# Attention and two token/channel mixers on one core: plain first pair in each chunk, attention's tail takes over splits

## The reference

```python
# attention, B=2, H=8, S=768, D=64, 16 clusters: q and k meet only where
# their nearest centroids agree
scores = np.where(mask, scale * (q @ k.T), -1e9)
x = softmax(scores) @ v                       # -> (B, S, 512)
# mixer 1: U (768,32), V (32,768), w_ch1 (512,2048), w_ch2 (2048,512)
u = x + (x.T @ U @ V).T
x = u + relu(u @ w_ch1) @ w_ch2
# mixer 2: w_tok1 (768,256), w_tok2 (256,768), w_ch1 (512,1536), w_ch2 (1536,512)
u = x + (relu(x.T @ w_tok1) @ w_tok2).T
out = u + relu(u @ w_ch1) @ w_ch2             # (2, 768, 512) float32
```

## Time and profile before

| | us |
|---|---|
| median of 3 runs | 819.98 (818.78 to 821.72) |
| the profiled execution | 820.13 |
| its span, first to last instruction | 818.2 |
| PE busy in the span | 767.1 (94%) |
| DVE, ACT, POOL busy | 579.1, 386.0, 234.2 |
| mean granted clock of TensorE | 0.97 |

### The profile page before, as it was taken

How to read it: one execution, slowest core, us unless ns; L and a number is a source line. 1 busy time by engine, 2 the same in 40 slices (tenths; PEclk the granted TensorE clock), 3 DMA queues, 4 the chain that set the end, 5 groups by cost and what they waited for, 6 DMA issues and landing times.

```text
span 818.2 us, 12517 instructions
## 1 busy us (share of the span) xinstructions
PE 767.1 (94%) x4165; PEld 684.9 (84%) x4165; DVE 579.1 (71%) x893; ACT 386.0 (47%) x698; POOL 234.2 (29%) x262
## 2 busy tenths in 40 slices
PE   7989999999999757999999799999979999979998
PEld 6878999999998546888888588888868898868987
DVE  5678999999998897556558656556694556585554
ACT  5568888888886532232236322232450242442320
POOL 1342233223348881221112511221051221103100
PEclk9999999999999967999999899999998999999999
DMA  8935444443530402212210112212110212033002
GB/s 252 203 107 141 98 120 110 106 119 98 127 89 1 155 26 78 78 52 67 88 52 1 52 52 78 78 52 68 35 52 28 76 52 78 26 131 100 27 26 77
DMA packets 64042, 66.64 MB, mean 81 GB/s; under 512 B 6400, under 2 KB 53824, under 8 KB 64000
## 3 DMA queue, kind: packets, MB, share of 16 engines
q1 hardware_dynamic: 64000, 66.09, 28.9%
HBM read 42.27 MB, written 4.72 MB: 57 GB/s over the span
## 4 chain that ended last, share of the span: by engine, by line
PE 56%; DVE 8%; issue 3%; POOL 0%; ACT 0%; ACTq 0%
PE bank L1101 28%; PE bank L1087 23%; PE bank L1053 3%; DVE bc_lo L1279 2%; DVE h L1299 1%; PE bank L1069 1%; DVE a_lo L1245 1%; DVE kT_hi L1303 1%; DVE x L1258 1%; DVE x L1253 1%; DVE moving_sum L1273 1%; PE bank L1038 0%; POOL kT_hi L979 0%; DVE w_lo L1284 0%; DVE kT_hi L1289 0%
## 5 line engine op out<-in xcount | busy, mean ns | idle before, releaser
L1182 ACT ACTIVATE qT_hi<-h 128x768 fp32r<-128x768 f32 x56 | 47.4, 846 | 303.8 <-DVE h L1299 245.1
L1087 PE MATMUL bank<-bc_hi,a_hi 128*128 128x384 f32 x392 | 136.1, 347 | 18.2 <-DVE bc_lo L1279 12.8
L1087 PE MATMUL bank<-bc_lo,a_hi 128*128 128x384 f32 x392 | 135.3, 345 | 0.0
L1087 PE MATMUL bank<-bc_hi,a_lo 128*128 128x384 f32 x392 | 134.4, 343 | 0.0
L1101 PE MATMUL bank<-w_hi,kT_hi 128*128 128x512 f32 x336 | 133.7, 398 | 0.0
L1101 PE MATMUL bank<-w_lo,qT_hi 128*128 128x512 f32 x336 | 133.0, 396 | 0.0
L1101 PE MATMUL bank<-w_hi,qT_hi 128*128 128x512 f32 x336 | 132.6, 395 | 0.0
L1299 DVE TENSOR_TENSOR h<-bank,h 128x384 f32<-128x384 f32 x140 | 75.0, 552 | 51.3 <-PE bank L1087 51.2
L969 POOL TENSOR_TENSOR a_raw<-a_raw 128x256 f32<-128x256 f32 x28 | 24.3, 868 | 285.1 <-DMA a_raw<-in_moe_w_ch_dram 285.1
L1289 DVE SCALAR_TENSOR_TENSOR kT_hi<-h,qT_hi 128x768 fp32r<-128x768 f32 x56 | 59.4, 1061 | 64.6 <-ACT qT_hi L1182 64.6
L595 DVE TENSOR_TENSOR pT_lo<-back,pT_hi 128x384 fp32r<-128x384 f32 x192 | 98.0, 551 | 6.7 <-ACT pT_hi L496 3.3
(11 more groups left out here) (144 smaller groups left out, 1380.1 us busy)
## 6 DMA issues: line engine op xcount, KB each, us to landing
a_raw<-in_moe_w_ch_dram SPq DMA_DIRECT2D x56, 256.0 KB, 3.2
w_raw<-in_moe_w_ch_dram SPq DMA_DIRECT2D x56, 256.0 KB, 2.7
Q<-qT_hi SPq DMA_DIRECT2D x64, 96.0 KB, 2.2
K<-kT_hi SPq DMA_DIRECT2D x64, 96.0 KB, 2.1
q_raw<-in_q_dram SPq DMA_DIRECT2D x8, 384.0 KB, 5.8
k_raw<-in_k_dram SPq DMA_DIRECT2D x8, 384.0 KB, 6.7
Q<-qT_lo SPq DMA_DIRECT2D x32, 96.0 KB, 2.1
K<-kT_lo SPq DMA_DIRECT2D x32, 96.0 KB, 2.1
```

Source lines behind the costliest of these rows:

```text
L1087: last = nc.tensor.matmul(up_bank(n, q), w[n % 2][:, A_SLOT[q], kt, :], y[:, q, kt, :], start=(kt == 0 and i == 0), stop=(kt == 1 and i == 2))
L1182: nc.scalar.activation(hs_hi[:, e, :], h[:, e, :], ACT.Relu).then_inc(hs_hi_made, 1)
```

## The change

The first pair of each chunk no longer uses the seven products. It is computed as four groups (i, k), one for each half of h. A group is 12 matmuls of 384 columns into one bank (`group`), over the plain blocks of the weights and of the tokens. ACT and DVE apply relu and split straight from that bank (`group_high`, `group_low`). The plain token blocks are split straight from the bank of the transposition (`block_high` on ACT, `block_low` on DVE), before `uT_copy` copies the tile to uT. The sums over uT and their splits (`t_block`, `t_high`, `t_low`) are needed only from pair 1 on. The first pairs need no `pair_sums`.

In attention, GpSimd splits three token tiles of sequence 0 in each of the pairs 5 and 6. In the last pair it splits U, V, and the columns of the first three head pairs of the six tiles of sequence 1. SP loads the weights of the pairs 0 and 1 once the last heads are in. PE ends attention with the 12 matmuls of the first token product of sequence 0. The mixers' block then only splits the last 128 columns of the six tiles of sequence 1. The loads and splits of wt1 and wt2 move from its start into the pairs 1 and 2 of chunk 0. In mixed chunks `token_second` moves behind product 1 of pair 1. The temporaries of the sums lie in h, and the raw token weights in uT.

```diff
@@ attention, SP: at the end
+            for j in range(2):
+                sp.wait_ge(head_in[j], NPAIR * HEAD_LOADS)
+            w3 = w_ch1.rearrange("(k p) f -> p k f", p=P)
+            for n in range(2):
+                for i in range(2):
+                    sp.dma_start(a_raw[n][:, 2 * i:2 * i + 2, :, :].rearrange("p s k c -> p (s k) c"),
+                                 w3[:, :, (2 * n + i) * P:(2 * n + i + 1) * P]).then_inc(w1_in[n], 16)
@@ attention, GpSimd
...
                     if last_pair:
                         if G == 0:
+                            for j in range(2):
+                                pool.wait_ge(head_in[j], NPAIR * HEAD_LOADS)
                             pool.wait_ge(uv_in, 5 * 16)
                             split_U()
-                        for i in range(2 * G, min(2 * G + 2, NT)):
-                            split_x(i)
+                        elif G == 1:
+                            split_V()
+                        else:
+                            if G == 2:
+                                pool.wait_ge(x_done, (NPAIR - 1) * GPP)
+                            for i in range(GT * (G - 2), GT * (G - 1)):
+                                split_x(1, i)
@@ attention, PE: at the end
+            U_st = q_lo[:, 0, :].rearrange("p (t c) -> p t c", t=NT)
+            pe.wait_ge(exp_done, NPAIR * TPP)
+            pe.wait_ge(U_split, 4)
+            pe.wait_ge(x0_split, 2 * NT)
+            for t in range(NT):
+                for n in range(2):
+                    last = nc.tensor.matmul(front[:, 0:DM], U_st[:, t, :], token_tiles(hi[n])[:, t, :],
+                                            start=(t == 0 and n == 0), stop=(t == NT - 1 and n == 1))
+            last.then_inc(tok_mm, 1)
@@ mixers, PE
+            def group(cc, g):
+
+                n, (i, k) = pbase[cc], GROUPS[g]
+                pe.wait_ge(b_made, cc * NT + NT // 2 * (k + 1))
+                if g == 0:
+                    pe.wait_ge(a_made, 2 * (n + 1))
+                if g < 2:
+                    pe.wait_ge(uT_made, cc * NT + (g + 1 if cc == 0 else NT - 1 + g))
+                else:
+                    pe.wait_ge(group_made, 4 * cc + g - 1)
+                for j in range(2):
+                    for kt in range(2):
+                        for c, (w, y) in enumerate(((a_hi, bc_hi), (a_hi, bc_lo), (a_lo, bc_hi))):
+                            last = nc.tensor.matmul(ring_bank(cc, g)[:, 0:GW], w[n % 2][:, 2 * i + j, kt, :],
+                                                    y[:, 5 * k + j, kt, :], start=(j == 0 and kt == 0 and c == 0),
+                                                    stop=(j == 1 and kt == 1 and c == 2))
+                last.then_inc(group_mm, 1)
...
             for cc in range(NCH):
-                for p in range(npair[cc]):
-                    for q in range(PRODS):
+                for g in range(len(GROUPS)):
+                    if cc == 0 and g < 2:
+                        for t in range(GT):
+                            transpose_u(0, GT * g + t)
+                    group(cc, g)
+                    if cc == 0 and g > 0:
+                        for t in range(2 * g - 2, 2 * g):
+                            token_second_low(1, t)
+                    if cc in MIXED:
+                        for t in ((), (0,), (1, 2), (3, 4, 5))[g]:
+                            token_first(cc, t)
+                for p in range(1, npair[cc]):
+                    for q in range(BLOCKS):
                         product(cc, p, q)
+                        if cc in MIXED and p == 1 and q == 1:
+                            for t in range(NT):
+                                token_second(cc, t)
@@ mixers, ACT
+            def block_high(cc, t):
+                act.wait_ge(u_tr, cc * NT + t + 1)
+                nc.scalar.activation(split_tile(bc_hi, t), turned(cc, t), ACT.Copy).then_inc(b_hi_made, 1)
+
             def uT_copy(cc, t):
-                act.wait_ge(u_tr, cc * NT + t + 1)
...
+                act.wait_ge(b_made, cc * NT + t + 1)
+                nc.scalar.activation(uT[:, :, t * P:(t + 1) * P], turned(cc, t), ACT.Copy).then_inc(uT_made, 1)
...
+                else:
+                    for t in range(NT):
+                        block_high(cc, t)
+                        if t > 0:
+                            uT_copy(cc, t - 1)
+                    uT_copy(cc, NT - 1)
...
+                    t_high(cc, 0)
+                    t_high(cc, 1)
+                    group_high(cc, 0)
+                    a_high(n + 1)
+                    t_high(cc, 2)
+                    group_high(cc, 1)
@@ mixers, DVE
+                dve.wait_ge(uT_made, NT * (cc + 1))
+                t_block(tmp2, block_of(0, 1), block_of(0, 0))
+                dve.wait_ge(t_sum, 4 * cc + 1)
+                t_block(tmp1, block_of(1, 1), tmp2)
+                t_block(block_of(0, 1), block_of(1, 1), block_of(0, 1))
...
+                    t_low(cc, 0)
+                    t_low(cc, 1)
+                    group_low(cc, 0)
+                    for part in range(2):
+                        a_low(n + 1, part)
+                    t_low(cc, 2)
+                    group_low(cc, 1)
+                    settle(cc, 0)
+                    settle(cc, 1)
+                    w2_low(n)
+                    group_low(cc, 2)
+                    settle(cc, 2)
+                    settle(cc, 3)
+                dve.wait_ge(t_made, 4 * cc + 1)
+                t_block(tmp1, block_of(1, 0), tmp1)
+                group_low(cc, 3)
+                if not mixed:
+                    settle(cc, 4)
+                    settle(cc, 5)
+                t_low(cc, 3)
```

More of the change, by code:

```diff
@@ new lines, in _ @@
+                for half in range(2):
+                    for t in range(GT * half, GT * half + GT):
+                        if cc == 0:
+                            add_mix(0, t)
+                    for t in range(GT * half, GT * half + GT):
+                        block_low(cc, t)
+                dve.wait_ge(uT_made, NT * (cc + 1))
+                t_block(tmp2, block_of(0, 1), block_of(0, 0))
+                dve.wait_ge(t_sum, 4 * cc + 1)
+                t_block(tmp1, block_of(1, 1), tmp2)
@@ new lines, in _ @@
+                dve.wait_ge(t_made, 4 * cc + 1)
[5 more added lines that the diff above has]
+                t_low(cc, 3)
+                if mixed:
+                    for r in range(NR):
+                        t2_low(cc, r)
+                for n in range(pbase[cc] + 1, pbase[cc + 1]):
+                    more = n + 1 < PAIRS_ALL
+                    combine(n, 1, c11, snap)
+                    if mixed and n == pbase[cc] + 1:
```

559 lines of the change are left out of this document (292 added, 267 removed).

## The result

| | before | after |
|---|---|---|
| median (lowest to highest, runs) | 820.63 us (818.78 to 821.72, 4) | 806.98 us (805.07 to 808.34, 4) |
| the profiled execution, its span | 820.13, 818.2 | 807.81, 806.0 |
| PE busy, mean granted clock | 767.1, 0.970 | 760.1, 0.989 |

The ratio is 0.9834, with a 95% interval of 0.9805 to 0.9864. The kernel is 13.7 us faster; the forecast was 806.0.

The account below looks back on a forecast made before the run. A steady-state pair was taken as bound by PE: its matmul columns, waits and clock. Terms of 11.7 (start and pair 1), 2.0, 2.0 and -1.6 summed to 14.1 off 820.13, giving 806.0 us, range 801 to 810.

Parts of the forecast that it names:

- Part 1: First pair of each chunk: four groups of 12 matmuls, 48 instead of 42, +1.04 us in each of four chunks.
- Part 2: Attention's last pair: GpSimd's added splits fit with 0.5 us slack, taken as 0; mixers start at 269.3 instead of 268.2.
- the list of signs: Trace marks for right or wrong; wrong included attention ending after 267 or chunk 0's first group later than 284.
- Part 3: Start of chunk 0: first down unit at 307.5 against 318.22, a gain of 10.7 us; 11.7 with pair 1.
- pair 1's loss at half clock: Chunk 0, pair 1: it had lost 2.1 us at half clock; 1.0 of that was kept as gain.
- the term that I priced 0: Chunk 0, pairs 1 and 2: wt1 and wt2 splits, 11 us on GpSimd beside VectorE work, cost nothing.
- Part 4: Transposition ring, chunks 1 to 3: 1.93 us a step, so downs end 4.0 us later at each of three boundaries.
- the rival: Clock falls in the transposition ring: 2.9 us lost at each of three boundaries, 814.7 us in all; chance 0.22.
- Part 5: After the ring: chunk 3 gains 2.4, chunks 1 and 2 6.0 each; less 4.0, a 1.6 loss and 2.0 gains.
- The sum: Whole kernel: 11.7 + 2.0 + 2.0 - 1.6 = 14.1 us faster, giving 806.0.

Follow-up runs that it names:

- changed again: The changed kernel itself, unedited, profiled a second time in another session; its span was 803.7 us, against 806.0 in the first profile.
- e2: Changed kernel with GpSimd splitting the second half of w_tok2 one pair later, in pair 3 of chunk 0; 804.69 us against 806.98.
- e9: Changed kernel with the edits of e1_ring and e2 together, without the other order of the blocks; 797.85 us against 806.98.
- e1_ring: Changed kernel with ScalarE copying each transposed tile right behind its high part, bank freed after VectorE's low part, chunks 1 to 3; 801.01 us against 806.98.
- e5: Changed kernel with VectorE doing additions and group low parts earlier in chunks 0 and 3, and sums pair 1 needs later; 809.13 us against 806.98.

## Why the prediction was right, point by point

**Part 1, the work of a group.** The 12 matmuls of group 0 in chunk 3 take 2.12 us in the chain, as two products do. Right.

**Part 2, attention's end.** Right, at a slack that was hardly larger than told (GpSimd's last finishes, with the idle time ahead):

```profile
265.02 0.82 POOL L410 TENSOR_TENSOR qT_hi<-x,zero 128x384 fp32r<-128x384 f32 x1
265.92 1.01 POOL L413 TENSOR_TENSOR kT_hi<-x,qT_hi 128x384 fp32r<-128x384 f32 x1
...
269.05 0.60 POOL L394 TENSOR_TENSOR avsum<-av 128x192 f32<-128x192 f32 x1 [0.92 <-ACT av L537]
```

A narrow tile takes 1.86, for which I had 1.9, and GpSimd idles 0.92 us before the last finish. Attention's own length is 202.82 against 202.86. That it ended 2.4 later in this execution came from the stretch ahead of it. By the list of signs this ("attention ending after 267", "a first group later than 284") would have stood for wrong: it was 268.5 and 284.3, for a reason that lies ahead of what was changed. A sign should be a distance between two marks, not a place in the span.

**Part 3, chunk 0.** The step that was mis-sized. From attention's last copy (266.08 before) I had the first group after 16.2 us and the first down unit after 41.4; three executions whose clock stayed up in the token product (changed again, e2, e9) have 14.2 and 37.5, the profiled one 15.8 and 39.4. The gain of this stretch was thus 12.7, and 14.6 in those three, where 10.7 was told. PE in the profiled execution:

```profile
284.32 0.44 PE L1157 MATMUL bank<-bc_hi,a_hi 128*128 128x384 f32 x1 [1.73 <-DVE bc_lo L1395]
...
289.36 0.41 PE L1157 MATMUL bank<-bc_hi,a_hi 128*128 128x384 f32 x1 [1.37 <-ACT uT L1259]
...
296.51 0.66 PE L1157 MATMUL bank<-bc_hi,a_hi 128*128 128x384 f32 x1 [3.91 <-DVE kT_hi L1411]
...
307.89 0.39 PE L1193 MATMUL bank<-w_hi,qT_hi 128*128 128x512 f32 x1
```

Two terms were too high in all four. The low part of the 768 late columns took 1.47 and not 1.9. And of the groups 2 and 3, group 2 alone ran at 1.2 GHz, behind the 3.91 us wait that I had foreseen, while group 3 was back at 2.4 GHz. The 12 matmuls of sequence 1's token product took the 4.1 told there, and 2.9 in "changed, again" (272.91 to 275.77). The stretches of sequence 1's token product, of group 2 and of what follows it:

```profile
273.90:281.10 7.20, 7.18 (x24) 5.70 (x25) 4.45 (x6) 0.60 (x1) 2.23 (x2) 0.76 0.20 69
...
296.50:301.00 4.50, 4.18 (x12) 3.68 (x12) 4.10 (x6) 2.79 (x6) 0.00 (x0) 0.50 0.00 0
301.00:305.00 4.00, 3.92 (x17) 3.62 (x18) 4.00 (x7) 0.22 (x1) 0.00 (x0) 0.80 0.38 128
```

The first of them is what separates the executions: in this one the clock fell to 1.2 GHz amid the token product (0.76 over the stretch). In "changed, again", at the same place, it didn't:

```profile
272.90:280.10 7.20, 7.05 (x36) 5.79 (x36) 5.25 (x7) 1.57 (x3) 2.22 (x2) 1.00 0.40 125
```

The wait ahead of it is the same 2.71 us in both. Which of the two a run gets isn't settled by anything I measured; it costs 1.6 us ahead of the first group here, and 2.9 in e1_ring (0.57 over its token product).

I had kept 1.0 of pair 1's loss at half clock. All of it went: 13.72 us from unit 0 to the next pair, where it was 15.6.

The error on the other side is the term that I priced 0: the wt2 splits beside VectorE's low parts. I had allowed for a doubling and found 0.4 us to spare. I had also put the splits of wt1 and wt2 at 11 us together; GpSimd was busy 6.2 us with the first and 9.4 with the second in the changed kernel. w2_low took 3.37 instead of 1.28 and a_low's first part 3.26 instead of 1.21, 2.6 and 2.7 times as much, and pair 2 took 17.23 us (321.61 to 338.84 in the chain) instead of the 15.6 that a pair takes. That is the +1.6 that e2 took away. The Trainium skill (SBUF — State Buffer, "Who interferes with whom") says that a VectorE instruction with two inputs in SBUF contends with a GpSimd instruction that reads SBUF, and that the one which comes second is blocked until the other is through. The trace agrees. a_low starts at 329.93 beside a GpSimd operation that ends at 332.11 (329.53 + 2.58); 332.11 plus its lone 1.21 is 333.3, and it ended at 333.19. w2_low is two instructions. The first meets the last 0.8 us of the 2.25 operation, the second, which the chain has at 327.89, the last 1.6 us of the CAST; 1.28 + 0.8 + 1.6 is 3.7, and it took 3.37. So what is added is the rest of the GpSimd operation that is met, and a doubling was the wrong picture of it.

**Part 4, the ring.** Right in mechanism and size. A step took 1.89 (1.93 told), T2 waited 1.74 (about 2 told), T0 to T5 took 9.15 instead of 5.23, +3.9 (4.0 told), all of it on the path (e1). The waits before T3 to T5 show as 0.58 and not 0.8 to 0.9, since the modelled end of a matmul lies past the start of the next work. The clock is the rival's point. The three rings of the changed kernel (boundaries 3, 2 and 1):

```profile
688.00:698.00 10.00, 6.53 (x40) 4.63 (x38) 4.37 (x7) 5.67 (x10) 0.27 (x1) 1.00 0.00 0
568.00:578.00 10.00, 6.54 (x37) 4.55 (x37) 4.35 (x7) 5.67 (x10) 0.00 (x0) 1.00 0.00 0
414.00:429.50 15.50, 12.53 (x61) 9.63 (x60) 6.44 (x9) 7.99 (x14) 0.00 (x0) 0.89 0.00 1
```

It stayed at 2.4 GHz in two and fell for a part of the third, which costs 0.9 us (T0 to T5 10.06). Which boundary has it changes from execution to execution, and some have none. In e1's shorter ring it fell in none. By the rule that I had cited from the Trainium skill (TensorE: Matmul & The Clock Gate, "Part 4: PE-mode transpose"), that a transposition does not count as activity for the clock, it would have fallen in all three, the rival priced at 2.9 each. It did not here; but no run had a ring of transpositions alone, so the rule itself is left as it was.

**Part 5, after the ring.** In chunk 3 I counted 15.0 from the end of the downs to the first unit; it was 14.7 (703.53 to 718.23), where it had been 17.4. With the ring, boundary 3 lost 1.2 (1.6 told). In chunks 1 and 2 token_second starts without its wait and warm, and add_mix's tail is exposed, as told. The chain, and PE's first down unit behind it:

```profile
451.95 8.44 PE bank L1124 x36
```

```profile
461.25 0.47 PE L1193 MATMUL bank<-w_hi,qT_hi 128*128 128x512 f32 x1 [0.87 <-DVE x L1380]
```

8.44 stands against 10.51 in the earlier trace rows, and the 5.4 us of "issue" ahead of it are gone. Boundary 2 gained 2.1 (2.0 told); boundary 1 gained 0.8, 1.65 in executions without the fallen clock.

**The sum.** Told: 10.7 + 1.0 + 2.0 + 2.0 - 1.6 = 14.1. Measured in the profiles: 12.7 + 1.9 - 1.6 + 0.8 + 2.1 - 1.2 = 14.7. Less 0.1 for the stretches that hardly differ and 2.4 for the stretch ahead of attention's first copy that is the 12.2 between the spans; the medians are 13.7 apart. The total is closer than its parts, and that is luck. Four errors of 1 to 2 us cancelled: the start (+2.0) and pair 1 (+0.9) brought more than told, the splits of wt2 (-1.6) and boundary 1 (-1.2) less.

## What to carry to other kernels

When an edit fills a hole in one engine's queue with what was late, ask what stands behind the moved instruction: e5 moved a sum on VectorE that nobody needed soon, and ScalarE's in-order queue made product 2 wait for it; moving one instruction of ScalarE behind the bank's release gave 3 us back. A ring of two banks is as fast as the reader that frees a bank last, so let the reader that needs the data least urgently not be that one. VectorE work with two SBUF inputs that has a few us of slack isn't free beside GpSimd: price each such instruction with up to the full length of the GpSimd instruction that it can meet.

## What was unexpected in the hardware

The granted clock of the same code, after the same waits, differs from one execution to the next: 0.76 or 1.00 in the token product behind a wait of 2.71 us, and a fall that costs 0.9 us in one ring of three, not always the same one. Beside GpSimd's splits VectorE's subtractions rose from 1.2 to 3.3 us, and its sums from 0.96 to between 1.4 and 2.8, depending on what they met. The stretch ahead of attention's first result varied by 5.4 us (63.2 to 68.6) over the profiled executions, more than most of the effects measured here; only the distance between marks tells effects of 1 to 2 us apart.
